# A recurrence with an MLP beside it: the MLP starts one slot later, and loads, scalings and one decay change their order

## The chip, the cores and the metric

One core of a Trainium2 chip. The metric is the device time of one execution in microseconds; the kernel before has a median of 1185.76 us over 3 runs (1184.65 to 1189.53).

## The reference

For each of 32 (batch, head) pairs a state of 40 x 40 runs over 768 tokens; its outputs, gathered to 3072 tokens of 320 values, go through two MLPs.

```python
for t in range(S):                      # S = 768, D = 40, B*H = 32
    y[:, :, t] = einsum('bhd,bhde->bhe', rt, state)
    Sa = einsum('bhde,bhe->bhd', state, at)
    state = state * wt[:, :, None, :] - einsum('bhd,bhe->bhde', Sa, bt) + einsum('bhd,bhe->bhde', vt, kt)
x = y as (3072, 320)
h = x @ w_in; g = maximum(0.01 * h, h); x = g @ w_out              # 320 -> 2048 -> 320
out = (sigmoid(x @ w_gate) * (x @ w_val)) @ w_out                   # 320 -> 1536 -> 320
```

All is float32; the products of the MLPs are made from a high and a low part of each operand.

## The kernel before

**The recurrence** is done in chunks of 64 tokens. A unit `u` (12 of them) holds two chunks, `n = 2u` and `n = 2u+1`; the index `c` is the chunk of a unit (in the layouts it separates two sets of sequences). For each chunk VectorE makes the running product of w (`dve_decay`: a scan into `decay`, then a reciprocal into `inv`, which has three buffers), GpSimd scales k and b by `inv` and a by `decay` (`pool_k`, `pool_b`, `pool_a`), and TensorE multiplies a with b (`"a"`) and a with k (`"ka"`) in `pe_a_ka`. A triangular matrix per chunk is inverted column by column on VectorE (`inverse_first`, `inverse_columns`), two units ahead of its use; it goes through DRAM to be laid out anew (`store_p`, `load_p`, `store_t`, `load_t`). With the inverse, TensorE, ScalarE and VectorE go through a fixed chain for each chunk: `rhs`, `first`, `cross`, `ut_u`, `st` (new state), `vrur`, `y`.

**The first MLP** runs beside it on TensorE in 96 steps `m` of one tile of 128 hidden values for a block of 128 tokens x 4 batches (6 blocks, 16 steps each). A step is `up_products(m)` (8 matmuls of 128x128 by 512), on ScalarE `act_g` (activation, then the rounded high part `g_hi`), on VectorE `dve_g_low` (the low part `g_lo`), and `down_products(m)` (8 matmuls), which is issued in the step after. At the start of a block, `act_x` and `dve_x` split the x block in high and low parts; at its end `act_o` copies three banks out and `store_o` stores them. Behind the recurrence the steps are alone on TensorE; then comes the second MLP, which also is dense.

**The order** is written by hand: every engine's program is a loop over windows `g` from -2 to 14 with eight slots `s` each. In window `g` the chunks `2g` and `2g+1` go through their chain (`now`), unit `g+1` is prepared (`soon`), unit `g+2` is begun (`later`). `mlp_step(g, s)` gives the step of a slot, `m = 8g + s - LAG`, so each slot has one MLP step ahead of its part of the recurrence. TensorE's slots: 0 `rhs, sn, first`; 1 `cross, a_ka, ut_u`; 2 `st, vrur`; 3 `rhs, y, first` (second chunk's rhs, first chunk's y); 4 `cross, a_ka, ut_u, sn`; 5 `st, vrur`; 6 `y`; 7 `kb`. Semaphores count each tile's readers and writers. `inv` for chunk `n` waits until b and k of chunk `n-3` are scaled; `dve_decay(n+5)` stands at the start of slot 1, `dve_decay(n+6)` in slot 6.

**SP** issues all loads and stores of the recurrence from one queue, in the order of `sync_program`, and waits there for the tile to be free; `load_late` holds v, r and `v_nu` (four DMAs), `load_k` waits for `pe_kb` (slot 7). x blocks are stored to DRAM by `store_y` and come back by `load_x`; both chunks' stores must have landed. `x_f`, the tile of x, is also the place of `vrur` and `u_feat`. GpSimd issues the loads of the weights; those of the second MLP wait for the last `store_y`.

Of the kernel before, what the change touches and what calls it, by code (L numbers as in the profile page):

```python
# [18 lines left out]
NJ = S // P  # L19
# [11 lines left out]
DN = 2 * DM  # L31
LAG = 17


def rwkv_mlp_kernel(nc, wF, aF, bF, kF, rF, vF, vT, vN, w_in, w_out1, w_gate, w_val, w_out2, out):
# [5 lines left out]
    with ExitStack() as ctx:  # L41
# [282 lines left out]
        def gpsimd_program(pool):  # L324
            constants(pool)
            for g in range(-2, NU):
                if unit_in(g + 1):
                    pool_k(pool, 2 * (g + 1))
                    pool_k(pool, 2 * (g + 1) + 1)
                if unit_in(g + 2):  # L330
                    for c in range(2):
                        pool_b(pool, 2 * (g + 2) + c)
                        pool_a(pool, 2 * (g + 2) + c)
                if g == -1:

                    pool.wait_ge(p_loaded, 32)
                    for i in range(4):
                        load_piece(pool, i)
                if g == 0:
                    for i in range(4, 8):  # L340
                        load_piece(pool, i)
# [138 lines left out]
        def sync_program(sp):  # L480
# [24 lines left out]
            for g in range(NU):  # L505
                n = 2 * g
                load_k(sp, g + 1)
                load_b(sp, g + 2)
                load_a(sp, n + 5)
                if g >= 4 and g % 2 == 0:  # L510
                    store_o(sp, g // 2 - 2)
                load_w(sp, n + 6)
                store_p(sp, n + 4)
                store_y(sp, n)
# [8 lines left out]
                if g % 2 == 1:  # L523
                    load_x(sp, g // 2)
                load_late(sp, g + 1)

# [280 lines left out]
        def tensor_program(pe):  # L807
            pe.wait_ge(constants_set, CONSTANTS)
            pe.wait_ge(vector_set, VECTOR_SET)
            for g in range(-2, NU + 3):  # L810
                for s in range(8):
                    m = mlp_step(g, s)
                    if m is not None:
                        up_products(pe, m)
                        if m > 0:
                            down_products(pe, m - 1)
                    now, soon, later = unit_in(g), unit_in(g + 1), unit_in(g + 2)
                    n = 2 * g
                    if s == 0 and now:
# [28 lines left out]
                    elif s == 5 and now:  # L848
                        pe_st(pe, n + 1)
                        pe_vrur(pe, n + 1)  # L850
                    elif s == 6 and now:
                        pe_y_begin(pe, n + 1)
                        pe_y_end(pe, n + 1)
                    elif s == 7 and soon:
# [157 lines left out]
        def scalar_program(act):  # L1012
            for g in range(-2, NU + 3):
                for s in range(8):
                    m = mlp_step(g, s)
                    n = 2 * g
                    if m is not None:
                        act_g(act, m)
                    if s == 0 and g % 2 == 0 and 1 <= g // 2 <= NJ:
                        act_x(act, g // 2 - 1)  # L1020
# [5 lines left out]
                    elif s == 1:  # L1026
                        if now:
                            act_cross(act, n)
                        if g >= 4 and g % 2 == 0 and g // 2 - 2 < NJ - 1:
                            act_o(act, g // 2 - 2)  # L1030
                        if later:
                            act_a(act, n + 4)
                        if now:
                            act_u(act, n)
                            act_ut(act, n)
                    elif s == 3 and now:
                        act_rhs(act, n + 1)
# [193 lines left out]
        def vector_program(dve):  # L1231
            dve_constants(dve)
            for g in range(-2, NU + 3):
                now, soon, later = unit_in(g), unit_in(g + 1), unit_in(g + 2)
                n = 2 * g
                for s in range(8):
# [4 lines left out]
                    elif s == 0 and soon:  # L1241
                        inverse_columns(dve, g + 1, 7, 12)
                    elif s == 1:
                        if later and n + 5 >= 4:
                            dve_decay(dve, n + 5)
                        if soon:
                            inverse_columns(dve, g + 1, 12, 14)
                    elif s == 2 and soon:
# [7 lines left out]
                    if m is not None:  # L1256
                        dve_g_low(dve, m)
                    if s == 0 and g % 2 == 0 and 1 <= g // 2 <= NJ:
                        dve_x(dve, g // 2 - 1)
                    if s == 1 and soon:  # L1260
                        dve_ka(dve, n + 2)
                    elif s == 2 and now:
# [116 lines left out]
```

## Time and profile before

| | |
|---|---|
| median of 3 runs | 1185.76 us |
| the profiled execution | 1187.38 us, span 1185.6 us |
| mean granted TensorE clock | 0.949 |
| TensorE busy | 1054.4 us, 89% |
| VectorE busy | 638.7 us, 54% |
| ScalarE busy | 384.7 us, 32% |
| GpSimd busy | 106.2 us, 9% |
| windows 0 to 11 of the recurrence | up to about 717 us |
| MLPs alone | from about 717 us to the end |

A busy share is a mean over regions with different limits; the stretches of single windows say which engine sets their length. Times are from the span's start. In a timeline the bracket behind a row is the idle time of that engine before it and who ended it.

### The profile page before, as it was taken

The numbers are of one execution on the slowest core, as the hardware profiler recorded it, in microseconds if no ns is written. First come the engines' busy times: TensorE is split into PE (matmuls) and PEld (weight loads), VectorE is DVE, ScalarE is ACT, GpSimd is POOL, SyncE is SP. The second block draws the span as 40 slices with busy tenths as digits, with TensorE's granted clock in tenths as the row PEclk, the third lists the DMA queues.
The fourth block names the chain that finished last, engine by engine and source line by source line (L and its number), as shares of the span: only waits on it lengthen the run. The fifth ranks groups of instructions, "written<-read, shape, count | busy, mean of one in ns | idle before, by whom it ended". The sixth has DMA issues, their size and how long they took to land.

```text
span 1185.6 us, 35874 instructions
## 1 busy us (share of the span) xinstructions
PE 1054.4 (89%) x15840; PEld 899.3 (76%) x15840; DVE 638.7 (54%) x1292; ACT 384.7 (32%) x746; POOL 106.2 (9%) x99
## 2 busy tenths in 40 slices
PE   2346659998999899999999997999999999999998
PEld 1345658777878687877778785888888888888887
DVE  7797776867687668685955222434323232322322
ACT  1122323334333433343343333543222222222322
POOL 5020210102020202020200000000000000000000
PEclk9986658998999899999999998999999999999999
DMA  5628261526243533444252204321010102010000
GB/s 175 202 92 213 76 176 37 153 50 185 60 142 77 165 74 116 102 141 124 73 133 64 61 9 136 110 94 45 1 59 1 58 1 58 1 58 1 23 1 23
DMA packets 134985, 99.79 MB, mean 84 GB/s; under 512 B 96560, under 2 KB 111920, under 8 KB 134832
## 3 DMA queue, kind: packets, MB, share of 16 engines
q1 hardware_dynamic: 132384, 85.06, 26.2%
q0 software_dynamic: 2448, 12.45, 3.0%
q8 instruction: 125, 2.05, 0.7%
q14 instruction: 28, 0.23, 0.1%
HBM read 78.61 MB, written 18.87 MB: 82 GB/s over the span
## 4 chain that ended last, share of the span: by engine, by line
PE 48%; issue 36%; DVE 7%; POOL 4%; DMA 3%; SPq 1%; ACT 1%; POOLq 0%; ACTq 0%; DVEq 0%
PE bank L781 11%; PE pair L781 11%; PE bank L730 6%; PE bank L801 4%; PE bank L799 4%; PE bank L800 4%; DVE prod L1127 2%; DVE t_unit L1131 2%; POOL a_sb L284 2%; PE bank L745 1%; DVE inv L1106 1%; PE bank L746 1%; PE bank L747 1%; POOL k_sb L298 1%; DMA x_f<-x 1%
## 5 line engine op out<-in xcount | busy, mean ns | idle before, releaser
L1176 DVE TENSOR_TENSOR g_lo<-g_full,g_hi 128x512 fp32r<-128x512 f32 x168 | 118.3, 704 | 213.1 <-ACT g_hi L945 212.9
L730 PE MATMUL bank<-x_hi,w_up 128*128 128x512 f32 x480 | 139.1, 421 | 13.1 <-ACT x_hi L954 8.2
L945 ACT CAST g_hi<-g_full 128x512 fp32r<-128x512 f32 x168 | 104.4, 621 | 134.7 <-DVE g_full L1228 131.6
L938 ACT ACTIVATE g_full<-bank 128x512 f32<-128x512 f32 x96 | 57.4, 598 | 245.3 <-PE bank L730 237.8
L1127 DVE TENSOR_TENSOR prod<-t_unit,p_unit 128x126 f32<-128x126 f32 (+22 forms) x372 | 106.6, 287 | 27.1 <-DMA p_unit<-p_dram 15.4
L1131 DVE TENSOR_TENSOR t_unit<-t_unit,prod 128x126 f32<-128x126 f32 (+22 forms) x372 | 109.9, 295 | 12.8
L730 PEld LDWEIGHTS bank<-x_hi,w_up 128*128 128x128 f32 x480 | 86.0, 192 | 32.9 <-ACT x_hi L954 8.6
L553 PE MATMUL bank<-a_sb,b_sb 40*64 40x64 f32 x768 | 35.2, 257 | 61.6 <-POOL a_sb L284 48.8
L1106 DVE RECIPROCAL inv<-decay 128x512 f32<-128x512 f32 x24 | 80.5, 3353 | 16.5 <-POOL k_sb L298 15.8
L1228 DVE TENSOR_TENSOR g_full<-pair,h_sb 128x512 f32<-128x512 f32 x36 | 24.9, 691 | 112.8 <-PE pair L781 112.1
L730 PE MATMUL bank<-x_lo,w_up 128*128 128x512 f32 x288 | 85.3, 406 | 0.0
L745 PE MATMUL bank<-g_hi,w_dn 128*128 128x512 f32 x192 | 77.4, 403 | 5.0 <-DVE g_lo L1176 5.0
L553 PEld LDWEIGHTS bank<-a_sb,b_sb 40*64 40x64 f32 x768 | 31.8, 167 | 63.6 <-issue 62.5
L298 POOL TENSOR_TENSOR k_sb<-k_sb,inv 128x512 f32<-128x512 f32 x24 | 33.8, 1428 | 475.8 <-DMA k_sb<-in_kF 475.8
L746 PE MATMUL bank<-g_hi,w_dn 128*128 128x512 f32 x192 | 76.3, 397 | 0.0
L1228 DVE TENSOR_TENSOR g_full<-bank,h_sb 128x512 f32<-128x512 f32 x36 | 24.9, 691 | 94.7 <-PE bank L781 86.3
L747 PE MATMUL bank<-g_lo,w_dn 128*128 128x512 f32 x192 | 75.7, 394 | 0.0
L730 PEld LDWEIGHTS bank<-x_lo,w_up 128*128 128x128 f32 x288 | 56.7, 197 | 13.0
L781 PE MATMUL pair<-x_hi,up 128*128 128x512 f32 x240 | 62.8, 391 | 0.0
L781 PE MATMUL bank<-x_hi,up 128*128 128x512 f32 x240 | 62.8, 391 | 0.0
L801 PE MATMUL bank<-dn,g_lo 128*128 128x320 f32 x192 | 59.3, 309 | 0.0
L800 PE MATMUL bank<-dn,g_hi 128*128 128x320 f32 x192 | 59.3, 309 | 0.0
(136 smaller groups left out, 2354.4 us busy)
## 6 DMA issues: line engine op xcount, KB each, us to landing
b_sb<-in_bF SPq DMA_DIRECT2D x12, 512.0 KB, 7.2
a_sb<-in_aF SPq DMA_DIRECT2D x24, 256.0 KB, 4.3
k_sb<-in_kF SPq DMA_DIRECT2D x12, 512.0 KB, 7.0
p_unit<-p_dram SPq DMA_DIRECT2D x24, 256.0 KB, 3.8
v_sb<-in_vF SPq DMA_DIRECT2D x12, 512.0 KB, 5.0
r_sb<-in_rF SPq DMA_DIRECT2D x12, 512.0 KB, 6.9
w_raw<-in_wF SPq DMA_DIRECT2D x20, 260.0 KB, 4.0
stage<-in_w_out POOLq DMA_DIRECT2D x7, 640.0 KB, 6.2
```

What stands on the lines that cost most here:

```text
L730: last = nc.tensor.matmul(up_bank(m)[:], lhs, rhs, start=(e == 0), stop=(e == len(products) - 1))
L745: nc.tensor.matmul(bank[1 + kk][:], w_high, hi, start=(f == 0), stop=False)
L746: nc.tensor.matmul(bank[1 + kk][:], w_low, hi, start=False, stop=False)
L747: nc.tensor.matmul(bank[1 + kk][:], w_high, lo, start=False, stop=(f == NF1 - 1))
L781: last = nc.tensor.matmul(o[:], lhs, rhs, start=(x == 0), stop=(x == len(products) - 1))
L800: nc.tensor.matmul(o, g_hi[:, par, tok], wt[:, 1, f % GT], start=False, stop=False)
L801: last = nc.tensor.matmul(o, g_lo[:, par, tok], wt[:, 0, f % GT], start=False, stop=(f == NF2 - 1))
L945: nc.scalar.copy(g_hi[:, m % 2], g_full[:]).then_inc(g_hi_ready, 1)
L1106: nc.vector.reciprocal(inv[:, n % 3], decay[:, n % 6, :, 1:L + 1]).then_inc(inv_ready, 1)
L1127: nc.vector.tensor_tensor(terms, t_unit[:, 0:m, t:t + 1].to_broadcast([P, m, rest]), p_unit[:, t, t + 1:C].unsqueeze(1).to_broadcast([P, m ...
L1131: nc.vector.tensor_tensor(t_unit[:, 0:m, t + 1:C], t_unit[:, 0:m, t + 1:C], terms, ALU.add).then_inc(column_ready, 1)
L1176: nc.vector.tensor_tensor(g_lo[:, m % 2], g_full[:], g_hi[:, m % 2].bitcast(F32), ALU.subtract).then_inc(g_lo_ready, 1)
```

## The change

Five things. `LAG` goes from 17 to 18: every MLP step, with `act_x`, `dve_x` and `act_o`, is one slot later (`act_o` stands in slot 2 after the chain's work). In slot 6 TensorE issues `y` between `up_products` and `down_products`. GpSimd scales chunk by chunk: k, b, a of one, then of the other. SP issues k and b of a window first, and v, r, `v_nu` behind them (in the window that uses them, no longer at the end of the one before); `store_o` goes behind `load_w` and `store_p`. `dve_decay(n+5)` moves from the start of VectorE's slot 1 to its end, behind `dve_g_low`, `dve_x` and `dve_ka`.

```diff
--- before.py
+++ after.py
@@ -29,7 +29,7 @@
 M2 = NJ * NF2
 MX = P // 2
 DN = 2 * DM
-LAG = 17
+LAG = 18
 
 
 def rwkv_mlp_kernel(nc, wF, aF, bF, kF, rF, vF, vT, vN, w_in, w_out1, w_gate, w_val, w_out2, out):
@@ -324,11 +324,10 @@
         def gpsimd_program(pool):
             constants(pool)
             for g in range(-2, NU):
-                if unit_in(g + 1):
-                    pool_k(pool, 2 * (g + 1))
-                    pool_k(pool, 2 * (g + 1) + 1)
-                if unit_in(g + 2):
-                    for c in range(2):
+                for c in range(2):
+                    if unit_in(g + 1):
+                        pool_k(pool, 2 * (g + 1) + c)
+                    if unit_in(g + 2):
                         pool_b(pool, 2 * (g + 2) + c)
                         pool_a(pool, 2 * (g + 2) + c)
                 if g == -1:
@@ -506,11 +505,13 @@
                 n = 2 * g
                 load_k(sp, g + 1)
                 load_b(sp, g + 2)
+                if g > 0:
+                    load_late(sp, g)
                 load_a(sp, n + 5)
+                load_w(sp, n + 6)
+                store_p(sp, n + 4)
                 if g >= 4 and g % 2 == 0:
                     store_o(sp, g // 2 - 2)
-                load_w(sp, n + 6)
-                store_p(sp, n + 4)
                 store_y(sp, n)
                 load_v_tok(sp, g + 1)
                 load_a(sp, n + 6)
@@ -522,7 +523,6 @@
                 store_y(sp, n + 1)
                 if g % 2 == 1:
                     load_x(sp, g // 2)
-                load_late(sp, g + 1)
 
             store_o(sp, NJ - 2)
             load_x2(sp, 0)
@@ -810,12 +810,15 @@
             for g in range(-2, NU + 3):
                 for s in range(8):
                     m = mlp_step(g, s)
+                    now, soon, later = unit_in(g), unit_in(g + 1), unit_in(g + 2)
+                    n = 2 * g
                     if m is not None:
                         up_products(pe, m)
-                        if m > 0:
-                            down_products(pe, m - 1)
-                    now, soon, later = unit_in(g), unit_in(g + 1), unit_in(g + 2)
-                    n = 2 * g
+                    if s == 6 and now:
+                        pe_y_begin(pe, n + 1)
+                        pe_y_end(pe, n + 1)
+                    if m is not None and m > 0:
+                        down_products(pe, m - 1)
                     if s == 0 and now:
                         pe_rhs_begin(pe, n)
                         pe_rhs_end(pe, n)
@@ -848,9 +851,6 @@
                     elif s == 5 and now:
                         pe_st(pe, n + 1)
                         pe_vrur(pe, n + 1)
-                    elif s == 6 and now:
-                        pe_y_begin(pe, n + 1)
-                        pe_y_end(pe, n + 1)
                     elif s == 7 and soon:
                         pe_kb(pe, n + 2)
                         pe_kb(pe, n + 3)
@@ -1016,7 +1016,7 @@
                     n = 2 * g
                     if m is not None:
                         act_g(act, m)
-                    if s == 0 and g % 2 == 0 and 1 <= g // 2 <= NJ:
+                    if s == 1 and g % 2 == 0 and 1 <= g // 2 <= NJ:
                         act_x(act, g // 2 - 1)
                     now, soon, later = unit_in(g), unit_in(g + 1), unit_in(g + 2)
                     if s == 0 and now:
@@ -1026,13 +1026,13 @@
                     elif s == 1:
                         if now:
                             act_cross(act, n)
-                        if g >= 4 and g % 2 == 0 and g // 2 - 2 < NJ - 1:
-                            act_o(act, g // 2 - 2)
                         if later:
                             act_a(act, n + 4)
                         if now:
                             act_u(act, n)
                             act_ut(act, n)
+                    elif s == 2 and g >= 4 and g % 2 == 0 and g // 2 - 2 < NJ - 1:
+                        act_o(act, g // 2 - 2)
                     elif s == 3 and now:
                         act_rhs(act, n + 1)
                         act_first(act, n + 1)
@@ -1240,11 +1240,8 @@
                             dve_decay(dve, first)
                     elif s == 0 and soon:
                         inverse_columns(dve, g + 1, 7, 12)
-                    elif s == 1:
-                        if later and n + 5 >= 4:
-                            dve_decay(dve, n + 5)
-                        if soon:
-                            inverse_columns(dve, g + 1, 12, 14)
+                    elif s == 1 and soon:
+                        inverse_columns(dve, g + 1, 12, 14)
                     elif s == 2 and soon:
                         inverse_columns(dve, g + 1, 14, 17)
                     elif s == 3 and soon:
@@ -1255,10 +1252,13 @@
                         dve_decay(dve, n + 6)
                     if m is not None:
                         dve_g_low(dve, m)
-                    if s == 0 and g % 2 == 0 and 1 <= g // 2 <= NJ:
+                    if s == 1 and g % 2 == 0 and 1 <= g // 2 <= NJ:
                         dve_x(dve, g // 2 - 1)
-                    if s == 1 and soon:
-                        dve_ka(dve, n + 2)
+                    if s == 1:
+                        if soon:
+                            dve_ka(dve, n + 2)
+                        if later and n + 5 >= 4:
+                            dve_decay(dve, n + 5)
                     elif s == 2 and now:
                         dve_st(dve, n)
                         dve_vrur(dve, n)
```

## Rows read from the trace of the kernel before

**Rows 1.** The page, part 1: busy time of the engines.
```profile
PE 1054.4 (89%) x15840; PEld 899.3 (76%) x15840; DVE 638.7 (54%) x1292; ACT 384.7 (32%) x746; POOL 106.2 (9%) x99
```

**Rows 2.** Windows view, TensorE: stretch; us, busy (matmuls), granted clock, DMA share, GB/s.
```profile
108.50:188.90 80.40, 53.66 (x1435) 0.59 0.48 129
221.93:277.41 55.48, 51.68 (x1159) 1.00 0.35 90
277.41:335.67 58.26, 54.35 (x1159) 0.94 0.48 134
335.67:390.23 54.56, 51.58 (x1159) 1.00 0.35 91
390.23:449.75 59.52, 54.66 (x1158) 0.94 0.47 132
449.75:502.87 53.12, 51.42 (x1160) 1.00 0.36 93
502.87:561.57 58.70, 54.46 (x1158) 0.94 0.47 129
561.57:614.39 52.82, 51.22 (x1159) 1.00 0.32 86
614.39:668.07 53.68, 50.92 (x1095) 1.00 0.38 102
716.72:734.98 18.26, 10.06 (x33) 0.72 0.39 129
734.98:789.73 54.75, 54.75 (x242) 1.00 0.36 116
```

**Rows 3.** Waits, 221.93 to 721 us: us in total, times, longest us.
```profile
PE bank L553 <- POOL a_sb L284: 7.1, 6, 1.7
...
PE bank L745 <- DVE g_lo L1176: 5.0, 3, 1.8
PE bank L730 <- issue: 4.9, 4, 1.6
```

**Rows 4.** Waits, 100 to 189 us.
```profile
PE bank L553 <- POOL a_sb L284: 13.7, 2, 9.6
```

**Rows 5.** Windows view: slot 0, slots 1 and 2 of window 9; slot 5 of window 8.
```profile
561.57:568.28 6.71, 6.50 (x151) 1.00 0.82 272
568.28:581.63 13.35, 12.35 (x292) 1.00 0.12 30
542.48:549.76 7.28, 7.28 (x115) 0.77 0.51 83
```

**Rows 6.** Timeline of the SP queue, 500 to 510 us: start us, us.
```profile
500.59 0.94 SPq L454 DMA_DIRECT2D x_f<-x  x2
...
505.96 0.53 SPq L377 DMA_DIRECT2D k_sb<-in_kF  x1
506.59 0.38 SPq L370 DMA_DIRECT2D b_sb<-in_bF  x1
```

**Rows 7.** DMA view, 500 to 520 us: issues, KB, us to landing.
```profile
v_sb<-in_vF SPq DMA_DIRECT2D x1, 512.0 KB, 5.6
...
k_sb<-in_kF SPq DMA_DIRECT2D x1, 512.0 KB, 7.3
```

**Rows 8.** Timeline of GpSimd, 500 to 550 us.
```profile
513.37 2.51 POOL L298 TENSOR_TENSOR k_sb<-k_sb,inv 128x512 f32<-128x512 f32 x2 [48.97 <-DMA k_sb<-in_kF]
```

**Rows 9.** Timeline of VectorE, 509 to 522 us.
```profile
508.64 0.68 DVE L1176 TENSOR_TENSOR g_lo<-g_full,g_hi 128x512 fp32r<-128x512 f32 x1
...
514.77 3.35 DVE L1106 RECIPROCAL inv<-decay 128x512 f32<-128x512 f32 x1 [2.50 <-POOL k_sb L298]
...
518.44 1.26 DVE L1131 TENSOR_TENSOR t_unit<-t_unit,prod 128x133 f32<-128x133 f32 x1
```

**Rows 10.** The page, part 5: busy us, mean ns | idle before.
```profile
L945 ACT CAST g_hi<-g_full 128x512 fp32r<-128x512 f32 x168 | 104.4, 621 | 134.7 <-DVE g_full L1228 131.6
...
L1131 DVE TENSOR_TENSOR t_unit<-t_unit,prod 128x126 f32<-128x126 f32 (+22 forms) x372 | 109.9, 295 | 12.8
```


## The prediction

> **What bounds the kernel now.** I read the page first: one core, one execution of 1187.38 us around a span of 1185.6 us, TensorE busy 89% of it [rows 1]. Then the busy table by stretches, cut where the first MLP `up` product of a window starts, to see where TensorE is not busy [rows 2]. The reader is to see three regions. From window 3 to window 9 each window holds the same 1159 matmuls and 51.2 to 51.6 us of TensorE work at full clock, but lasts 52.8 to 59.5 us: even windows (4, 6, 8) are long, 58.3 to 59.5, with a granted clock of 0.94 in the mean, odd ones short. Windows 1 and 2 (their slots up to 188.9) are not bound by TensorE: 53.66 us busy in 80.40, clock 0.59. From 734.98 on the stream is dense: 54.75 us hold 242 matmuls, so a matmul costs 0.226 and one MLP step of 16 costs 3.62 us. Between the last window and that lies a stretch of 18.26 us with 10.06 busy: TensorE stands still for 8.2 us, for the last block of x, and its 33 matmuls take 10.1 instead of 7.5 us, 2.6 us lost to the clock that fell in that wait.
>
> Then the waits of TensorE inside the windows [rows 3]: 7.1 us for `a_sb` scaled by GpSimd, 5.0 us for `g_lo` of VectorE, 4.9 us ahead of L730 filed under "issue"; the L730 ones are the starts of new x blocks, because `dve_x` is late. These waits are only 17 us. The rest of the long windows is the clock: it falls to half (0.5, that is 1.2 instead of 2.4 GHz) around such idle pieces and all matmuls of the slot stretch. In windows 1 and 2 the `a_sb` wait alone is 13.7 us in two pieces [rows 4].
>
> What makes `a_sb` late is read in window 8, whose slot 0 starts at 502.87. SP issues the x block at 500.6, then v, r and `v_nu`, and k only at 505.96 and b at 506.59 [rows 6]; k lands 7.3 us later [rows 7], at 513.3. GpSimd scales two k tiles from 513.37, 1.26 us each [rows 8], then b and a. VectorE has stood before its reciprocal for 2.50 us until 514.77, since `inv` is free only when k is scaled, and `g_low` and `inverse_columns` are queued behind it [rows 9]. So one late k load holds TensorE (through `a_sb`), VectorE (through `inv`) and then TensorE again (through `g_lo`).
>
> **Loads of k and b ahead.** No DMA is added. k can go when `pe_kb` is done, which is slot 0's start, so in window 8 at about 502.9 instead of 505.96, with v, r, `v_nu` (1.35 MB of the 2.6 MB from x to k) behind it. v took 5.6 us in that queue where k took 7.3; I take 5.5 for k: it lands at T0+5.6 (T0 = slot 0's start), not T0+10.4. GpSimd in its new order needs k, b, a = 3.8 us and is done at T0+9.4; slot 0 lasts 6.71 [rows 5], `up`, `down` and `pe_cross` take 4.65 us more, so `pe_a_ka` wants it at T0+11.4: no wait, 2 us to spare. Bounds: 0 if k lands by T0+7.6; if the order changes nothing, k lands at T0+10.4, `a_sb` is ready at T0+14.2 and the wait is 2.8 us. v and r are late next: they and `v_nu` land when b does today, about T0+11.6, with `load_a(n+5)` behind them; `pe_st` in slot 2 wants `v_nu` at T0+17.3. Covered by nearly 6 us.
>
> **MLP one step later, act_x and dve_x in slot 1.** Today `dve_x` starts at 509.24, right after slot 0's inverse columns and `g_lo` at 508.64 [rows 9], and the new block's `up` is due at 509.6 and starts at 511.23. With the block one slot later, `dve_x` is due at T0+13.3 and can end at T0+12.9 (x_hi of slot 1 ready at T0+11.8): wait 1.6 us goes to 0 in windows 4, 6, 8 and 10. The three `act_x` passes of 0.62 us [rows 10] now stand ahead of `act_cross`, beside `down` and `pe_cross` (2.6 us): they cost at most 0.3. `act_o` in slot 2 has `pe_st`, `pe_vrur` and `up` (3.8 us) over its 1.6. `store_o` moves behind `load_w` and `store_p`; `dve_y` in slot 3 wants it some 3 us after it lands. All four of these at 0; uncovered, `act_o` would cost 1.6 in three or four windows.
>
> One step fewer lies beside the recurrence and one more is dense: +3.62 us dense, and window 2's slot 1 loses its `up`.
>
> **Decay(n+5) at the end of slot 1.** Its scan and reciprocal are 1.23 + 3.35 = 4.6 us. Ahead of `g_low` they made `down` wait (the 5.0 us). Behind `dve_ka` they start when `ka` is multiplied, T0+12.5, plus 0.7: done at T0+17.8. Then GpSimd scales b and a of chunk n+5, 2.5 us, and here a row speaks against the change: beside GpSimd's b, an addition on `t_unit` took 1.26 us [rows 9], where this line's mean is 0.295 [rows 10]; the reciprocal beside k did not stretch (3.35). So slot 2's six column operations take 1.95 + 1.5 = 3.4 us, `g_low` ends at T0+21.9, and slot 3's `down` wants it at T0 + 6.7 (slot 0) + 12.35 (the work of slots 1 and 2) [rows 5] + 1.95 (`up`) = T0+21.0. I charge 0.9 to 1 us in each of windows 3 to 9. Bounds: 0 if the two don't collide, 2.5 if every GpSimd operation blocks fully.
> The Trainium skill ("SBUF — State Buffer", Who interferes with whom) says that a VectorE instruction with two SBUF inputs and a GpSimd one exclude each other for a whole instruction. By that rule two GpSimd operations would cost up to 2.5 us instead of 1.5 and the seven windows 7 us more than my sum; the trace agrees on who is blocked, with 1.26 beside 0.29.
>
> **y between up and down in slot 6.** `pe_y_begin` and `pe_y_end` (2 us) and `down` swap; `y` ends 1.9 us earlier. Up to window 8 VectorE sits in `dve_decay(n+6)` then, so `dve_y` gains nothing. In windows 9 and 11 it does.
>
> **The sum.** Windows 3 to 10 today: 446.1 us in total [rows 2]. After: 51.4 of work, 0.4 that slot 4 has always before `pe_sn`, 1.0 for `g_low` = 52.8 for 4, 5, 6, 7 and 9. Window 3 gets 53.8 (GpSimd still beside slot 0's columns). Window 8 gets 54.2: its slot 5 at clock 0.77 took 7.28 instead of 5.7 (a slot of the same work is in the second row) after an idle piece before `pe_sn` that no edit touches [rows 5]; I keep about half. Window 10 loses only its 1.6: 52.0. Total 424.0, gain 22.1.
> Tail: the chain from the last `y` to x_lo is unchanged but starts 1.9 us earlier and has one step (3.6) more over it: 8.2 - 5.5 = 2.7 us of waiting. The 2.6 us of slow clock there I take at somewhat over half. Gain 5.5 + 1.5 = 7.0.
> Windows 1 and 2: of the 13.7 us, window 1 loses its wait of 9.6 down to where VectorE, continuously busy after the columns, takes over: I take 2.5 (bounds 0 and 6). In window 2 the x block stays in front of k and v, r, `v_nu` go behind it, so k lands some 4.5 us earlier, and the `rhs` copy no longer waits behind `act_x` for x; VectorE's slots 1 and 2 (columns, `dve_x`, `ka`, decay, columns: 13 us from there) follow at once. Slot 3 then starts at about 183.4 instead of 188.9, where the first row of [rows 2] ends: gain 5.5 (bounds 3 and 7; 4.1 is the whole rest of the 13.7).
> 22.1 + 7.0 + 8.0 - 3.6 = 33.5 us. Against its own 1187.4 the profiled time becomes 1153.9; the median of the runs is 1185.8, 1.6 lower, so 1152.3.
>
> **Rivals.** *The order of the loads gives little* (DMA shares its engines among queued transfers). For it: k and b, issued 0.6 apart after 1.35 MB, landed nearly together. Then windows 4, 6, 8 wait 2.8 us and lose 1.6 to the clock each (13), and windows 1 and 2 gain nothing (8): gain 12, 1174 us. Against it: v, first in the queue, took less than k. The Trainium skill ("DMA: Bandwidth & Descriptors", Queues, rings and completion order) says that one queue's descriptors start in ring order, though completion isn't ordered; the times 5.6 and 7.3 agree.
> *VectorE becomes the bound*: `g_low` in slot 3 is late by 3 us, not 1, and the clock falls with it (1.6): 3.6 x 7 = 25 us, 1177 us. For it: blocked operations; against it: VectorE is busy 54% of the span [rows 1], and only its order in slots 1 and 2 is tight.
> *Better than summed*: VectorE isn't late at all (7), window 1 gains 6 (3.5), the tail's slow step goes (1): 1141 us.
> *Slower*: v, r and `v_nu`, now behind k and b, are late for slot 2. Each us past T0+17.3 costs one in each of windows 1 to 10; the gain is gone from 3.4 us, that is landing at T0+20.7, nine later than I expect; four us more give 1192 or above. Against it: 2.4 MB moved by T0+11.6 today.
> *It does nothing*: the gained time is lost at other idle pieces with clock falls, 1186.
>
> **Chances and range.** Forecast 0.60 (own range 1146 to 1160), better 0.12, load order 0.11, VectorE 0.10, nothing 0.03, slower 0.04. The range 1143 to 1174 holds the forecast, most of the better case and the load rival. 0.5% is 6 us, about what this kernel's measurement tells from no change; all cases but the last two are beyond it: faster 0.93, same 0.03, slower 0.04.
>
> **What the profile after should show.** k landing before T0+7 and no `pe_a_ka` wait for `a_sb`; no L730 wait at a block's start in slot 2; even and odd windows of equal length, near 53; the reciprocal with no wait for k; a `g_lo` wait of about 1 us in slot 3; about 2.7 us before the last x block. A clock that still falls in every even window, or a wait of `pe_st` for `v_nu`, would make the prediction wrong.

## The result, and the profile after

| | before | after |
|---|---|---|
| median | 1185.2 us (4 runs, 1183.74 to 1189.53) | 1171.65 us (4 runs, 1168.31 to 1174.26) |
| ratio | | 0.9878, 95% interval 0.9842 to 0.9914 |
| profiled execution, span | 1187.38 us, 1185.6 us | 1168.31 us, 1166.6 us |
| mean granted clock | 0.949 | 0.988 |
| VectorE busy | 638.7 us | 662.4 us |

The change gains 13.6 us by the medians, where 33.5 were forecast. The profiled execution is the fastest of the four (the others were granted 0.956 to 0.969 of the clock), so against the profile before it shows 19.1 us of gain; below, that one is accounted for. Of the 5.5 us between the two gains, 2.2 are the profile before above its median and 3.3 this one below its own.

A column operation is one of the 744 small VectorE operations (lines L1127 and L1131) that invert the triangular matrices; each reads two tiles in SBUF. The page before has `t_unit`'s line in [rows 10]; the other half of the column operations is

```profile
L1127 DVE TENSOR_TENSOR prod<-t_unit,p_unit 128x126 f32<-128x126 f32 (+22 forms) x372 | 106.6, 287 | 27.1 <-DMA p_unit<-p_dram 15.4
```

The page after, the lines that answer to [rows 1] and to both halves:

```profile
PE 1045.6 (90%) x15840; PEld 890.4 (76%) x15840; DVE 662.4 (57%) x1292; ACT 384.9 (33%) x746; POOL 105.6 (9%) x99
...
L1127 DVE TENSOR_TENSOR prod<-t_unit,p_unit 128x126 f32<-128x126 f32 (+22 forms) x372 | 120.7, 325 | 27.9 <-DMA p_unit<-p_dram 16.2
...
L1131 DVE TENSOR_TENSOR t_unit<-t_unit,prod 128x126 f32<-128x126 f32 (+22 forms) x372 | 120.0, 323 | 12.8
```

VectorE does the same 1292 instructions and is busy 23.7 us longer. The mean of a column operation rose from 295 to 323 ns on L1131 and from 287 to 325 on L1127. Together the 744 operations take 240.7 instead of 216.5 us, which is all of the 24 us. It is not that each became a little longer: in windows 3 to 10 of the timelines, 18 column operations take over 1.1 us before and 39 after, and none lies between 0.5 and 1.1. The two behind the reciprocal in each of windows 3 to 9 stand in both; those ahead of it, in the columns of slots 0 and 1, went from 4 to 25.

The windows, cut as in [rows 2] (stretch; us, TensorE busy (matmuls), granted clock, DMA share, GB/s); window 3 starts at 215.69 here:

```profile
215.69:270.78 55.09, 51.72 (x1159) 1.00 0.40 107
270.78:325.45 54.67, 51.88 (x1159) 1.00 0.47 126
325.45:380.94 55.49, 51.95 (x1158) 1.00 0.42 106
380.94:435.54 54.60, 51.49 (x1160) 1.00 0.46 127
435.54:489.50 53.96, 51.73 (x1159) 1.00 0.42 109
489.50:545.31 55.81, 52.63 (x1159) 1.00 0.46 124
545.31:601.34 56.03, 51.90 (x1159) 1.00 0.37 100
601.34:652.37 51.03, 50.82 (x1094) 1.00 0.36 106
701.02:715.88 14.86, 12.75 (x50) 0.89 0.39 133
```

Windows 4, 6 and 8, which took 58.3 to 59.5 us, take 54.6 to 55.8, and no clock fall is left in them: the granted clock is 1.00 in every window from 3 to 10. But the odd ones hardly changed or got longer: 3 is 0.4 us shorter, 5 went from 54.56 to 55.49, 7 from 53.12 to 53.96 and 9 from 52.82 to 56.03. All stand 2 to 4 us above their 51.5 to 52.6 us of work. Slot by slot in window 9, against [rows 5]:

```profile
545.31:552.01 6.70, 6.49 (x150) 1.00 0.78 289
552.01:560.51 8.50, 6.89 (x181) 1.00 0.38 93
560.51:566.24 5.73, 5.73 (x119) 1.00 0.16 26
566.24:575.09 8.85, 7.81 (x183) 1.00 0.01 4
```

The rows are slots 0 to 3. The idle time is in slots 1 (1.61 us) and 3 (1.04 us). The waits after, as [rows 3], say for what:

```profile
POOL b_sb L291 <- DVE inv L1106: 63.9, 7, 11.2
...
PE bank L745 <- DVE g_lo L1176: 12.4, 10, 1.7
...
PE bank L553 <- issue: 0.5, 1, 0.5
```

The waits for `a_sb` (7.1 us) are gone, and of those at the start of a block (4.9) one of 0.8 is left in window 6; the wait of `down` for `g_lo` went from 5.0 us in three pieces to 12.4 in ten: 5.5 us in the slots 1 of windows 3, 5, 8 and 9, and 6.9 in the slots 3 of all windows from 3 to 9 but 7. Where `g_lo` is held up is read in slots 0 and 2 of window 9, which starts at 545.31. GpSimd:

```profile
548.95 1.27 POOL L298 TENSOR_TENSOR k_sb<-k_sb,inv 128x512 f32<-128x512 f32 x1 [37.55 <-DMA k_sb<-in_kF]
550.24 1.27 POOL L291 TENSOR_TENSOR b_sb<-b_sb,inv 128x512 f32<-128x512 f32 x1
551.47 1.21 POOL L284 TENSOR_TENSOR a_sb<-a_sb,decay 128x512 f32<-128x512 f32 x1
552.65 1.32 POOL L298 TENSOR_TENSOR k_sb<-k_sb,inv 128x512 f32<-128x512 f32 x1
565.12 1.28 POOL L291 TENSOR_TENSOR b_sb<-b_sb,inv 128x512 f32<-128x512 f32 x1 [11.15 <-DVE inv L1106]
566.35 1.25 POOL L284 TENSOR_TENSOR a_sb<-a_sb,decay 128x512 f32<-128x512 f32 x1
```

k is scaled from T0+3.6 (T0 is the start of the window's slot 0), and four scalings follow each other. VectorE in the same stretch is in its inverse columns:

```profile
548.68 0.28 DVE L1127 TENSOR_TENSOR prod<-t_unit,p_unit 128x115 f32<-128x115 f32 x1
548.99 1.36 DVE L1131 TENSOR_TENSOR t_unit<-t_unit,prod 128x115 f32<-128x115 f32 x1
550.39 1.25 DVE L1127 TENSOR_TENSOR prod<-t_unit,p_unit 128x110 f32<-128x110 f32 x1
551.68 1.14 DVE L1131 TENSOR_TENSOR t_unit<-t_unit,prod 128x110 f32<-128x110 f32 x1
552.85 1.27 DVE L1127 TENSOR_TENSOR prod<-t_unit,p_unit 128x126 f32<-128x126 f32 x1
554.15 0.29 DVE L1131 TENSOR_TENSOR t_unit<-t_unit,prod 128x126 f32<-128x126 f32 x1
...
554.99 0.68 DVE L1176 TENSOR_TENSOR g_lo<-g_full,g_hi 128x512 fp32r<-128x512 f32 x1
...
565.16 1.39 DVE L1131 TENSOR_TENSOR t_unit<-t_unit,prod 128x136 f32<-128x136 f32 x1
566.58 1.17 DVE L1127 TENSOR_TENSOR prod<-t_unit,p_unit 128x128 f32<-128x128 f32 x1
...
568.66 0.68 DVE L1176 TENSOR_TENSOR g_lo<-g_full,g_hi 128x512 fp32r<-128x512 f32 x1
```

The reader is to see the durations against the starts above: the operation at 548.68 takes 0.28 us, the four that meet a scaling take 1.36, 1.25, 1.14 and 1.27, the next is back at 0.29. Each of them ends 0.13 to 0.15 us after a scaling does. Below, this is called blocking. `g_lo`, in the queue behind them, comes at 554.99; `down` of slot 1 was due at 554.1. The same happens with two scalings behind the reciprocal, and slot 2's `g_lo`, which slot 3's `down` waits for, comes at 568.66.

### The profile page after: what moved, and what is told of

Same layout as the page of the kernel before. It is cut to its first block, busy times and chain, and to the rows that moved or that the text cites. A ratio compares the mean times of both kernels' runs of the same rounds, so it can differ in the third digit from the quotient of the medians.

```text
span 1166.6 us, 35874 instructions
## 1 busy us (share of the span) xinstructions
PE 1045.6 (90%) x15840; PEld 890.4 (76%) x15840; DVE 662.4 (57%) x1292; ACT 384.9 (33%) x746; POOL 105.6 (9%) x99
## 4 chain that ended last, share of the span: by engine, by line
PE 50%; DVE 2%; issue 0%; ACT 0%; ACTq 0%; DVEq 0%
PE bank L781 11%; PE pair L781 11%; PE bank L730 6%; PE bank L801 4%; PE bank L799 4%; PE bank L800 4%; PE bank L745 2%; PE bank L746 2%; PE bank L747 2%; PE bank L750 1%; PE bank L749 1%; DVE prod L1127 1%; DVE t_unit L1131 1%; PE bank L706 1%; PE bank L697 0%
## 5 line engine op out<-in xcount | busy, mean ns | idle before, releaser
L1176 DVE TENSOR_TENSOR g_lo<-g_full,g_hi 128x512 fp32r<-128x512 f32 x168 | 120.8, 719 | 212.2 <-ACT g_hi L945 212.2
L1127 DVE TENSOR_TENSOR prod<-t_unit,p_unit 128x126 f32<-128x126 f32 (+22 forms) x372 | 120.7, 325 | 27.9 <-DMA p_unit<-p_dram 16.2
L730 PE MATMUL bank<-x_hi,w_up 128*128 128x512 f32 x480 | 133.7, 408 | 2.9 <-issue 2.9
L938 ACT ACTIVATE g_full<-bank 128x512 f32<-128x512 f32 x96 | 57.4, 598 | 233.4 <-PE bank L730 189.5
L1131 DVE TENSOR_TENSOR t_unit<-t_unit,prod 128x126 f32<-128x126 f32 (+22 forms) x372 | 120.0, 323 | 12.8
L730 PE MATMUL bank<-x_lo,w_up 128*128 128x512 f32 x288 | 82.0, 393 | 0.0
L553 PEld LDWEIGHTS bank<-a_sb,b_sb 40*64 40x64 f32 x768 | 30.8, 163 | 52.3 <-issue 51.4
```

The source lines that it names most:

```text
L730: last = nc.tensor.matmul(up_bank(m)[:], lhs, rhs, start=(e == 0), stop=(e == len(products) - 1))
L1127: nc.vector.tensor_tensor(terms, t_unit[:, 0:m, t:t + 1].to_broadcast([P, m, rest]), p_unit[:, t, t + 1:C].unsqueeze(1).to_broadcast([P, m ...
L1131: nc.vector.tensor_tensor(t_unit[:, 0:m, t + 1:C], t_unit[:, 0:m, t + 1:C], terms, ALU.add).then_inc(column_ready, 1)
L1176: nc.vector.tensor_tensor(g_lo[:, m % 2], g_full[:], g_hi[:, m % 2].bitcast(F32), ALU.subtract).then_inc(g_lo_ready, 1)
```

## The experiments

Twelve kernels. Each was timed beside the kernel before on the same chip; ratios are to that. In a diff, lines with - are of the kernel named in the text. Two ratios whose intervals overlap are not told apart.

| run | what | median us | ratio, 95% interval |
|---|---|---|---|
| e1 | after, decay(n+5) back | 1185.79 | 0.9995 (0.9968 to 1.0022) |
| e2 | after, g_low ahead of columns | 1167.74 | 0.9838 (0.9787 to 0.9889) |
| e3 | after, seven eighths of the scaling left out | 1140.68 | 0.9617 (0.9557 to 0.9678) |
| e4 | before, MLP one step later alone | 1196.67 | 1.0102 (1.0071 to 1.0132) |
| e5 | after, v and r loads back | 1187.61 | 1.0004 (0.9975 to 1.0034) |
| e6 | before, order of loads alone | 1196.48 | 1.0096 (1.0065 to 1.0128) |
| e7 | e2, fewer meetings | 1159.06 | 0.9779 (0.9731 to 0.9828) |
| e8 | before, decay alone | 1192.19 | 1.0052 (1.0024 to 1.0080) |
| e9 | after, GpSimd's order back | 1172.91 | 0.9854 (0.9817 to 0.9892) |
| e10 | after, y back | 1174.34 | 0.9866 (0.9828 to 0.9904) |
| e11 | after, second k beside the reciprocal | 1165.71 | 0.9800 (0.9759 to 0.9841) |
| e12 | e7, state ahead of columns | 1151.11 | 0.9688 (0.9650 to 0.9725) |

### Is it GpSimd that holds the columns? e3

```diff
-            nc.gpsimd.tensor_tensor(t, t, inv[:, n % 3], ALU.mult).then_inc(k_scaled, 1)
+            nc.gpsimd.tensor_tensor(t[:, 0:1], t[:, 0:1], inv[:, n % 3, 0:1], ALU.mult).then_inc(k_scaled, 1)
```

and the same for b and a.

> The changed kernel, with GpSimd scaling only the first of eight column groups of a, b and k (seven eighths of the scaling are left out). Blocking: column operations beside GpSimd are back near 0.3 us, the waits for g_lo go, and windows 3 to 9 fall from 54.0 to 56.0 to about 52: 1150 us or less (GpSimd is also never late here). Rival 'position': slot 3 still waits about 1 us for g_lo in each window, 1160 to 1165 us.

Measured 1140.68 us, 31 below the changed kernel. Its page, and its windows 3, 7, 8 and 9:

```profile
L1127 DVE TENSOR_TENSOR prod<-t_unit,p_unit 128x126 f32<-128x126 f32 (+22 forms) x372 | 94.9, 255 | 27.8 <-DMA p_unit<-p_dram 16.1
L1131 DVE TENSOR_TENSOR t_unit<-t_unit,prod 128x126 f32<-128x126 f32 (+22 forms) x372 | 97.0, 261 | 12.8
```

```profile
203.05:255.02 51.97, 51.37 (x1158) 1.00 0.44 114
411.09:466.21 55.12, 51.72 (x1159) 1.00 0.42 106
466.21:520.25 54.04, 51.66 (x1159) 1.00 0.47 128
520.25:573.27 53.02, 51.76 (x1158) 1.00 0.41 106
```

The means are 255 and 261 ns, below those of before (287 and 295) too, and no column operation takes over 0.5 us, so blocking makes up 24.6 us of the 744 operations in the kernel before (216.5 - 191.9) and 48.8 in the one after (240.7 - 191.9). No wait for `g_lo` of 0.2 us or more is left between 215 and 700 us. Slot 3 doesn't wait, though the decay stands where the change put it: the rival "position" falls. Between the two profiled spans lie 28.0 us: 15.3 in windows 3 to 10, of which 5.3 in the slots 1 and 9.2 in the slots 3 of windows 3 to 9, and 12.6 before window 3, where k, b and a are also ready sooner; how those 12.6 divide is not shown.

One half of the expectation failed. Windows 3 to 6 last 51.8 to 52.2 us, but 7, 8 and 9 last 55.1, 54.0 and 53.0, with 3.4, 2.4 and 1.3 us idle and hardly any scaling to meet. Window 7 is longer here than in the changed kernel (53.96). So what keeps windows 7 to 9 above 52 us is in good part something else; it comes back below.

### Is it the queue behind the columns? e2

```diff
                     elif s == 0 and soon:
+                        if m is not None:
+                            dve_g_low(dve, m)
                         inverse_columns(dve, g + 1, 7, 12)
```

and likewise in slot 2 ahead of columns 14 to 17; the common `dve_g_low` is left out there.

> The changed kernel with dve_g_low put ahead of inverse_columns in slots 0 and 2; nothing else. Blocking: the columns stay as long as they are (about 10.6 us for the first twelve in odd windows instead of 6.7), but g_lo no longer queues behind them, so the waits of down for g_lo in slots 1 and 3 (12.4 us in ten pieces, and what follows them) go: 1150 to 1160 us. Rival 'VectorE has too much to do': the wait moves to the columns, the new state or y further on, 1168 to 1175 us.

The waits for `g_lo` fell from 12.4 to 0.7 us, as said, but the time by only 4 us (ratio 0.9838 against 0.9878, intervals that overlap), a miss of the 1150 to 1160 forecast and the edge of what the rival gave. The profile has 435.0 us in windows 3 to 10, where the changed kernel has 436.7. The blocked columns still stand ahead of `dve_x`, the new state and `vrur`: the blocks that start in windows 4 and 6 wait 0.8 and 1.1 us, and slot 3 of windows 3 to 9, but for 7, still lasts 8.0 to 9.2 us instead of 7.5, with up to 0.9 of it waiting for the state. So the waits moved, as the rival said; that VectorE has too much to do is not shown by it, since e12 takes them away with the same work.

### Fewer meetings: e11, e7, e12

e11 is the changed kernel with one wait more on GpSimd:

```diff
                 for c in range(2):
                     if unit_in(g + 1):
+                        if c == 1 and g >= 0 and unit_in(g + 2):
+                            pool.wait_ge(decay_ready, 2 * g + 6)
                         pool_k(pool, 2 * (g + 1) + c)
```

> The changed kernel with one wait more: GpSimd scales the second k tile when the scan of decay(n+5) is done, so beside the reciprocal instead of beside slot 0's columns. Blocking: each of the windows loses one blocked column operation (1 us of VectorE time, 8 us over the run), the g_lo wait of slot 1 falls from 1.6 to about 0.6 us: 3 to 7 us faster than the changed kernel, 1165 to 1169. Rival 'the scalings' place does not matter, only g_low's': no difference, 1171.

Measured 1165.71 us, 6 us below the changed kernel by the medians and 9 by the ratios (0.9800 against 0.9878, intervals that just don't overlap). VectorE is busy 653.6 us, 8.8 less than after (one blocked operation of 1 us in each of eight windows had been forecast), windows 3 to 10 last 432.2 instead of 436.7 us, and the `g_lo` waits fall from 12.4 to 7.9 us. Nothing but the moment of one scaling changed, so the meeting itself costs. Not each window lost one blocked column operation: in windows 3 to 10 they fall from 39 to 35, since the scalings that stay meet other columns than before.

e7 puts e2 and e11 together and moves the decay ahead of `dve_ka` in odd windows:

```diff
                     if s == 1:
+                        if g % 2 == 1 and later and n + 5 >= 4:
+                            dve_decay(dve, n + 5)
                         if soon:
                             dve_ka(dve, n + 2)
-                        if later and n + 5 >= 4:
+                        if g % 2 == 0 and later and n + 5 >= 4:
                             dve_decay(dve, n + 5)
```

> The changed kernel with dve_g_low ahead of the columns in slots 0 and 2 as in e2, and fewer meetings of GpSimd and VectorE: GpSimd scales the second k tile only when the scan of decay(n+5) is done, so beside the reciprocal, and in odd windows the decay stands before dve_ka, in VectorE's idle time. Blocking: about 1 us less of columns in slot 0, 1.2 us less lateness in slot 3 of odd windows: 5 to 10 us below e2's 1167.7, 1157 to 1163 us. Rival 'throughput of VectorE': 1165 to 1170.

1159.06 us, as expected. Windows 3 and 5 last 51.8 and 52.1 us; 7 to 9 last 54.3, 56.5 and 53.5.

e12 is e7 with the columns of slot 2 behind the state:

```diff
-                        inverse_columns(dve, g + 1, 14, 17)
+                        if not now:
+                            inverse_columns(dve, g + 1, 14, 17)
...
                         dve_st(dve, n)
                         dve_vrur(dve, n)
+                        if soon:
+                            inverse_columns(dve, g + 1, 14, 17)
```

> e7 with slot 2's columns behind dve_st and dve_vrur. In e7 slot 3 of window 6 still waits 0.8 us for the state and slots 3 of the even windows last 8.0 to 9.0 instead of 7.5 us; that goes: 1 to 3 us below e7's 1159.1. If VectorE is simply full, the wait moves to g_lo of slot 3 and the time stays at 1158 to 1161.

1151.11 us, a larger gain than expected. Of the 7.5 us between the two profiled spans, only 2.1 lie in windows 3 to 10, which is inside the 1 to 3 expected; 4.1 come before window 3, which I hadn't looked at, and about 1.3 from a clock fall less at the last x block. Whether the state's place earned those 5.4 us or they are the spread of the clock is open. It is the best version: 37 us below the kernel before on the same chip (1188.5 us), 0.9688, where the change alone has 0.9878.

```profile
211.72:636.46 424.74, 412.95 (x9159) 1.00 0.43 116
```

These are its windows 3 to 10: 424.7 us, where the prediction had 424.0 for the change. And 23 column operations are still blocked in them, all ahead of the reciprocal, where the change has 25. So blocked columns cost little by themselves; they cost what is queued behind them and TensorE waits for.

### Which part of the change carries it: e4, e6, e8 alone; e1, e5, e9, e10 undone

e4 is the kernel before with `LAG = 18`, `act_x` and `dve_x` in slot 1, `act_o` in slot 2 and `store_o` behind `store_p`:

```diff
-LAG = 17
+LAG = 18
...
-                    if s == 0 and g % 2 == 0 and 1 <= g // 2 <= NJ:
+                    if s == 1 and g % 2 == 0 and 1 <= g // 2 <= NJ:
                         dve_x(dve, g // 2 - 1)
```

> The kernel before with only the MLP one slot later and what goes with it (act_x, dve_x in slot 1, act_o in slot 2, store_o later). By my step of the prediction: the 1.6 us wait at the start of a block goes in windows 4, 6, 8 and 10, and 3.6 of the 8.2 us before the last block go, but the late k stays: 1172 to 1178 us. Rival (the moved x block alone brings nothing, the late k does it all): 1183 to 1187 us.

A miss of both ranges: 1196.67 us, 11 slower. Its waits in the windows:

```profile
PE bank L553 <- POOL a_sb L284: 14.0, 6, 4.4
...
DVE inv L1106 <- POOL k_sb L298: 12.1, 3, 4.5
```

TensorE gets to `pe_a_ka` sooner and waits there for the late k all the longer (7.1 us in six pieces before, 14.0 in six now, the longest 4.4), and `dve_x`, now in slot 1, stands behind a reciprocal that waits for k.

e6 is the kernel before with only the order of loads:

```diff
                 load_b(sp, g + 2)
+                if g > 0:
+                    load_late(sp, g)
                 load_a(sp, n + 5)
...
-                load_late(sp, g + 1)
```

> The kernel before with only v, r and v_nu loaded behind k and b. By the prediction's step k lands some 4 us earlier in even windows and the waits for a_sb and of the reciprocal for k go, the 1.6 us for x stays: 1170 to 1176 us. Blocking: the scalings go over to slot 0's columns, so x_lo and g_lo are later by 2 to 4 us in every window: 1180 to 1190 us.

1196.48 us: not my prediction's step, but blocking, and more of it than said. In window 4 GpSimd, VectorE and TensorE:

```profile
277.96 1.71 POOL L291 TENSOR_TENSOR b_sb<-b_sb,inv 128x512 f32<-128x512 f32 x1
```

```profile
276.80 1.75 DVE L1177 TENSOR_TENSOR g_lo<-g_full,g_hi 128x512 fp32r<-128x512 f32 x1
278.47 3.93 DVE L1183 TENSOR_TENSOR x_lo<-x_f,x_hi 128x512 fp32r<-128x512 f32 x3
```

```profile
282.50 2.47 PE L731 MATMUL bank<-x_hi,w_up 128*128 128x512 f32 x5 [5.32 <-issue]
```

The three `x_lo` passes of window 8 before took half of that:

```profile
509.24 1.89 DVE L1182 TENSOR_TENSOR x_lo<-x_f,x_hi 128x512 fp32r<-128x512 f32 x3
```

The scalings now run from 275.5 on, `g_lo` takes 1.75 us instead of 0.68 and the `x_lo` passes 3.93 instead of 1.89, and `up` waits 5.32 us for them, with the granted clock falling to half in that wait. Here both sides are longer: the scaling at 277.96 takes 1.71 us. Such a wait stands in windows 4, 6, 8 and 10: 17.7 us in four pieces.

e8 is the kernel before with only `dve_decay(n + 5)` behind `dve_ka`.

```diff
                     elif s == 1:
-                        if later and n + 5 >= 4:
-                            dve_decay(dve, n + 5)
                         if soon:
                             inverse_columns(dve, g + 1, 12, 14)
...
                         if soon:
                             dve_ka(dve, n + 2)
+                        if later and n + 5 >= 4:
+                            dve_decay(dve, n + 5)
```

> The kernel before with only dve_decay(n+5) moved behind dve_ka in slot 1. The late k no longer holds VectorE with g_low behind it: 5.0 us of g_lo waits go, but pe_a_ka still waits for the late k in even windows, and slot 3 waits 1 to 1.7 us for g_lo in seven windows: 1180 to 1190 us. If the decay's place is what carries the gain by itself: 1172 to 1176.

1192.19 us by the median, 1.0052 by the ratio: slower by half a per cent, beyond the range I gave. Its `g_lo` waits rose to 7.0 us in seven pieces (six of them in slot 3, 1.0 to 1.1 each, the size that I had predicted for it), and the waits for the late k stayed (6.2 us).

So each of the three parts alone makes the kernel slower, and together they gain. (The change has two parts more, the order of the scalings and the place of `y`; e9 and e10 find nothing measurable in them.) Undone one at a time in the changed kernel:

```diff
                     elif s == 1:
+                        if later and n + 5 >= 4:
+                            dve_decay(dve, n + 5)
                         if soon:
                             inverse_columns(dve, g + 1, 12, 14)
...
                             dve_ka(dve, n + 2)
-                        if later and n + 5 >= 4:
-                            dve_decay(dve, n + 5)
```

> The changed kernel with one part undone: dve_decay(n+5) back at the start of VectorE's slot 1. Theory 'blocking' (a GpSimd scaling stops VectorE's two-input operations for its whole length, about 1 us each; four scalings now lie over slot 0's columns and two over slot 2's): the wait for g_lo in slot 3 (1.0 to 1.7 us in seven windows) goes, but g_lo of slot 1 comes behind 4.6 us of decay and columns that are still blocked, so slot 2 waits instead: 1166 to 1178 us, within 6 us of the changed kernel's 1171.7. Rival 'position' (only the later place of the decay costs, the columns of slot 0 do not matter): seven windows lose their 2 us, 1157 us or so.

e1, the decay ahead again, loses everything: 1185.79 us, above both ranges. The slot 3 waits go and slot 2 waits come, as said; what I missed is that `dve_x` is behind the decay as well, so `up` waits 4.2 to 5.1 us for a new block in windows 4, 6 and 8:

```profile
PE bank L730 <- issue: 14.3, 3, 5.1
...
PE bank L745 <- DVE g_lo L1176: 10.1, 7, 1.7
```

e5, `load_late` back at the end of the window before:

```diff
-                if g > 0:
-                    load_late(sp, g)
...
+                load_late(sp, g + 1)
```

> The changed kernel with the loads of v, r and v_nu back at the end of the window before, ahead of k. Load order matters (my prediction): k lands near 10 us behind slot 0's start in even windows again, pe_a_ka waits up to 3 us there, and windows 1 and 2 lose 5 to 8 us: 1180 to 1190 us. Rival 'order gives little': 1170 to 1175. Blocking says besides that slot 0's columns are free of GpSimd in even windows, so slot 1 waits for a_sb and no longer for g_lo.

1187.61 us, inside the range of the prediction's mechanism: the wait for `a_sb` is back with 13.4 us in three pieces (4.7 the longest, in windows 4, 6 and 8), and in those windows slot 1 has no wait for `g_lo`, as blocking says. The rival that the order of loads gives little falls, for the changed kernel; alone, in e6, the order gives nothing.

e9, GpSimd's order back (k, k, b, a, b, a), and e10, `y` back behind `down`:

```diff
-                for c in range(2):
-                    if unit_in(g + 1):
-                        pool_k(pool, 2 * (g + 1) + c)
-                    if unit_in(g + 2):
+                if unit_in(g + 1):
+                    pool_k(pool, 2 * (g + 1))
+                    pool_k(pool, 2 * (g + 1) + 1)
+                if unit_in(g + 2):
+                    for c in range(2):
```

> The changed kernel with GpSimd's order undone (k, k, b, a, b, a). Four scalings still lie in slot 0, so the columns stay as long; a and b of the first chunk are 1.3 us later, at about 9 us behind slot 0's start where pe_a_ka wants them at 11.4: no difference beyond 3 us, 1169 to 1174. If the new order carries part of the gain: over 1177.

```diff
-                    if s == 6 and now:
-                        pe_y_begin(pe, n + 1)
-                        pe_y_end(pe, n + 1)
...
                     elif s == 5 and now:
                         pe_st(pe, n + 1)
                         pe_vrur(pe, n + 1)
+                    elif s == 6 and now:
+                        pe_y_begin(pe, n + 1)
+                        pe_y_end(pe, n + 1)
```

> The changed kernel with y back behind down in slot 6. By the prediction it moves only the last x block: 1.9 us more of waiting there, 1171 to 1176. If y matters in every window: over 1177.

1172.91 and 1174.34 us, ratios 0.9854 and 0.9866 against 0.9878: neither can be told from the changed kernel.

## Why the prediction was wrong

The direction was right and the median lies in the range given; the gain was 40% of the forecast. By its terms, in the two profiled executions (us gained):

| term | predicted | measured |
|---|---|---|
| windows 1 and 2 (all before window 3) | 8.0 | 6.2 |
| windows 3 to 10 | 22.1 | 9.5 (446.1 to 436.7) |
| window 11 | 0 | 0 (48.65 both) |
| tail, less the dense step | 7.0 - 3.6 = 3.4 | 3.4 (18.26 for two steps to 14.86 for three) |
| sum | 33.5 | 19.1 |

**The step that failed** is the one that said "Window 3 gets 53.8 (GpSimd still beside slot 0's columns)" and gave the other windows nothing for it, though my own first step had just moved k to T0+5.6 and the end of k, b, a to T0+9.4, that is onto columns 7 to 12 in every window. Before, in window 8, k was scaled from 513.37 (T0+10.5) on, behind slot 0's columns, and the second k, b and a of the first chunk beside the reciprocal, which took its 3.35 us all the same. Measured: 25 blocked column operations ahead of the reciprocal in windows 3 to 10 instead of 4, and the slots 1 of windows 3 to 9 last 57.4 us together where 7 x 6.65 = 46.6 were taken and window 3 allowed one more: 9.8 us of the 12.6 that windows 3 to 10 fell short. Of the 10.8 above 46.6, 5.5 are `down` waiting for `g_lo`, 0.8 the x block in window 6, 0.5 `pe_a_ka` in window 4, 1.9 idle pieces in windows 7 and 8 that aren't GpSimd's (see **A term at nothing**), and the rest pieces below 0.3 us. Without most of the scaling (e3) these slots last 52.1 us, 5.3 less. e3 and e11 show that it is the scalings, e6 that the early k alone brings them there (18 instead of 4), and e12 that it is the order of VectorE's queue that makes them cost time.

**Slot 3** was nearly right. I charged 1.0 us of waiting for each of seven windows, 7.0 in all; the waits for `g_lo` there are 6.9 us, 1.0 to 1.1 in windows 3, 5 and 9, 1.7 in 4 and 6 (where `dve_x` stands ahead as well), 0.3 in 8 and none in 7. The slots as a whole last 62.2 us, 9.5 over 7 x 7.52; the other 2.6 are shorter pieces that were not read further. The rule of the Trainium skill ("SBUF — State Buffer", Who interferes with whom) that the prediction had set beside the sum, VectorE and GpSimd shutting each other out for a whole operation, would have made it 14 by the prediction's working, which did not come. For the single operation the trace agrees with it: the six blocked operations above are stretched from 0.3 to 1.14 to 1.39 us, each to the end of a scaling of 1.2 to 1.3, and the two behind the reciprocal cost VectorE 2.0 us where the sum took 1.5.

**A term at nothing**: beside what it charged for `g_low`, the prediction gave every full window 51.4 us of work and 0.4 of idle time, and only window 8 some more. Windows 7 to 9 have idle pieces of 0.5 to 2.0 us ahead of `ut_u` (slot 1 of 7 and 8) and of `ut_u` or `sn` (slot 4 of 8 and 9) in all the kernels with the MLP one step later, in e3 too, where these windows last 53.0 to 55.1 us without a blocked column. The profile before has such pieces in other places, the 1.43 us in window 8's slot 4 among them. A load of instructions starts 0.4 to 2 us before most of them, but such loads come every 4 to 8 us; that they cause the pieces was not tried and stays open.

**Windows 1 and 2**: window 2's slot 3 starts at 179.47 instead of 188.90, 9.4 us earlier against 8.0 predicted; its slots 3 to 7 then lose 3.2 us, with `down` waiting 2.2 us for `g_lo` behind the decay. The step missed that slot 3's lateness begins in window 2. And this is the fastest execution: in e9 and e10, which differ from the changed kernel in nothing that could be told in the time, window 3 starts at 219.0 and 218.8 us instead of 215.69, with more of the half clock before it. That is as much as this execution lies below the median; whether the unprofiled ones lost it there can't be seen.

**What was right**: k lands at T0+5.1 in window 8 (5.6 said) and at T0+3.6 in window 9; `pe_a_ka` waits for `a_sb` no longer; the wait at the start of x blocks is gone in windows 4, 8 and 10 and 0.8 in 6; v, r and `v_nu` are in time; the clock doesn't fall in windows 3 to 10 of this execution, and TensorE's work in windows 4, 6 and 8 fell by that from 163.5 to 156.0 us, 7.5 of the 11.4 that they gained; the 8.2 us wait ahead of the last block is 2.1 (2.7 said). `y` in slot 6 moves only the end: in e10 the wait ahead of the last block is 4.4 us instead of 2.1 (1.9 more were said), and windows 3 to 10 last 436.8 us.

**The rivals**: "VectorE becomes the bound" was the nearest in mechanism and too harsh in size (it would have put windows 3 to 9 at 4.6 us above 51.8; they stand 3.3 above it in the mean, and the clock falls did not come). "The order of the loads gives little" is refuted by e5. That v and r would be late did not show. e12, a different kernel, reaches what was forecast for the change (1151.11 against 1152.3); that is partly luck, since 5.4 us of it lie outside windows 3 to 10. That each part alone is slower was not among the rivals, and is the larger lesson: the gains depend on each other, and e4, e6 and e1 show how: k, x and the decay are served by one VectorE queue.

## What to carry to other kernels

When a transfer is made to land earlier, ask beside what its consumer will then run, as well as who was waiting for it: here the scalings left the reciprocal, which kept its 3.35 us beside them, for short two-input operations that each became 1 us longer. Put what TensorE waits for (`g_low`, the state) ahead of work that has time (the columns) before tuning anything else. And test the parts of a change alone and undone: three parts that each lose 0.5 to 1% gained 1.2% together, and with the queue in order 3.1%.

## What the runs showed of the hardware that was not expected

A GpSimd scaling of 1.25 us beside VectorE's short column operations was itself hardly stretched (1.21 to 1.32 us in window 9), while the column operation beside it grew from 0.28 to 1.14 to 1.39 us; leaving out seven eighths of the scaling took 31 us off the run. Beside a longer VectorE operation both grow: in e6 `g_lo` (0.68 us alone) and `x_lo` take 1.66 to 1.76 us and the scalings among them 1.56 to 1.75. The reciprocal took 3.35 us in the mean of every run, whatever stood beside it.

The four executions of the changed kernel had granted clocks of 0.988, 0.969, 0.966 and 0.956 and times of 1168.31, 1171.64, 1171.66 and 1174.26 us, so here the faster ones have the higher clock, over a spread of 0.5%. It is no rule: of the ten executions of e1 the one with the highest clock, 0.991, took 1188.09 us, and the fastest, 1179.38, had 0.957. Where the clock fell in the other three can't be seen; in the profiles of e9 and e10, whose spans are 4 and 7 us longer, most of the half clock lies between 90 and 204 us, in windows 0 to 2.
